# A three-block attention and mixture kernel on one core: new order of the steps inside an attention slot, masks behind both heads' scores, hi/lo splits as steps of their own

## What is computed

```python
# 1: attention, 8 heads of 64; heads 0-3 see the last 32 keys, heads 4-7 each 32nd key
scores = scale * q @ k.T ; masked ; attn = softmax(scores) ; x = attn @ v   # x: 576 x 512
# 2: token mixing and a channel layer
theta = x @ w_theta
yr = einsum('ts,bsd->btd', w_tok_r, x * cos(theta)) ; yi = the same with w_tok_i and sin
u = x + yr + yi ; x2 = u + relu(u @ w_ch)
# 3: 4 experts, top 2 by a gate, each a causal attention of one head
q, k, v = x2 @ wq[e], x2 @ wk[e], x2 @ wv[e]
out += gate[e] * (softmax(causal(q k.T)) @ v) @ wo[e]
```

## Time and profile before

| | us |
|---|---|
| median of 3 runs | 807.71 (800.57 to 808.68) |
| profiled execution | 807.49 |
| its span, first to last instruction | 805.7 |
| PE busy / DVE busy / ACT busy / POOL busy | 662.0 / 368.5 / 267.8 / 125.9 |
| one pass of BODY (third) | 193.7 |

### The profile page before, as it was taken

How to read it: one execution, slowest core, us unless ns; L and a number is a source line. 1 busy time by engine, 2 the same in 40 slices (tenths; PEclk the granted TensorE clock), 3 DMA queues, 4 the chain that set the end, 5 groups by cost and what they waited for, 6 DMA issues and landing times.

```text
span 805.7 us, 13113 instructions
## 1 busy us (share of the span) xinstructions
PE 662.0 (82%) x4469; PEld 535.7 (66%) x4469; DVE 368.5 (46%) x858; ACT 267.8 (33%) x791; POOL 125.9 (16%) x132
## 2 busy tenths in 40 slices
PE   3766798779888888787889879878888788997987
PEld 2654697768555588777655569767755558985654
DVE  2562755346546423355644633344554553334353
ACT  3461542453222441253421253044422145121222
POOL 1212330012201150012111133001120113100111
PEclk9695999999579998799866999889966899998769
DMA  7402044100000104200000011410000010000001
GB/s 237 116 18 78 11 99 99 31 16 16 1 1 0 53 9 109 50 4 20 8 1 1 27 34 35 94 31 15 18 1 0 1 40 21 1 1 1 1 1 59
DMA packets 73433, 27.33 MB, mean 34 GB/s; under 512 B 68624, under 2 KB 68624, under 8 KB 73360
## 3 DMA queue, kind: packets, MB, share of 16 engines
q1 hardware_dynamic: 70992, 22.70, 11.3%
q10 hardware_dynamic: 2368, 3.70, 1.2%
HBM read 21.67 MB, written 4.72 MB: 33 GB/s over the span
## 4 chain that ended last, share of the span: by engine, by line
PE 57%; issue 18%; DVE 10%; ACT 7%; POOL 4%; SPq 1%; DMA 1%; POOLq 0%; ACTq 0%; DVEq 0%
PE acc L1056 27%; PE wide L1056 11%; PE wide L1135 8%; PE turned L1170 4%; ACT probs L710 3%; POOL probs L648 2%; DVE xt L899 2%; PE turned L1155 2%; DVE probs L872 1%; ACT probs L718 1%; PE wide L1140 1%; DMA raw_k<-in_k 1%; PE wide L1116 1%; POOL probs L657 1%; DVE absf L914 1%
## 5 line engine op out<-in xcount | busy, mean ns | idle before, releaser
L727 ACT ACTIVATE pt<-turned 128x288 f32<-128x288 f32 (+5 forms) x72 | 30.8, 439 | 189.3 <-PE turned L1170 126.8
L1135 PE MATMUL wide<-k,q 64*128 64x128 f32 (+5 forms) x192 | 84.2, 592 | 0.6 <-DVE k L985 0.6
L1170 PE MATMUL turned<-ident,probs 128*128 128x128 f32 (+2 forms) x240 | 43.3, 324 | 41.6 <-DVE probs L872 26.4
L657 POOL TENSOR_TENSOR probs<-probs,weight 128x128 f32<-128x128 f32 (+4 forms) x40 | 31.5, 804 | 252.8 <-DVE weight L879 252.8
L840 DVE TENSOR_REDUCE nmax<-wide 128x1 f32<-128x128 f32 (+4 forms) x80 | 39.5, 537 | 56.8 <-PE wide L1140 56.7
L1170 PEld LDWEIGHTS turned<-ident,probs 128*128 128x128 f32 (+2 forms) x240 | 30.7, 172 | 50.6 <-DVE probs L872 24.5
L710 ACT ACTIVATE probs<-wide,nmax 96x128 f32<-96x128 f32 (+1 forms) x176 | 61.6, 379 | 5.7 <-DVE nmax L835 5.6
L1056 PE MATMUL wide<-w_tok_hi,z_hi 128*128 128x288 f32 x216 | 48.7, 307 | 11.1 <-POOL z_lo L673 11.1
L718 ACT ACTIVATE probs<-wide,nmax 128x128 f32<-128x128 f32 (+4 forms) x80 | 44.6, 573 | 26.0 <-DVE nmax L840 22.0
L666 POOL TENSOR_TENSOR xu_lo<-xt,xu_hi 128x576 fp32r<-128x576 f32 x16 | 22.5, 1403 | 162.3 <-ACT xu_hi L734 162.3
L1056 PE MATMUL wide<-w_tok_hi,z_lo 128*128 128x288 f32 x216 | 47.7, 303 | 0.0
(11 more groups left out here) (163 smaller groups left out, 1566.9 us busy)
## 6 DMA issues: line engine op xcount, KB each, us to landing
raw_q<-in_q SPq DMA_DIRECT2D x32, 128.0 KB, 2.4
raw_k<-in_k SPq DMA_DIRECT2D x32, 128.0 KB, 2.4
out<-o_sb SPq DMA_DIRECT2D x16, 256.0 KB, 2.0
raw_v<-in_v SPq DMA_DIRECT2D x64, 31.5 KB
raw_v<-in_v SPq DMA_DIRECT2D x16, 120.0 KB
raw_r<-in_moe_w_tok_r ACTq DMA_DIRECT2D x1, 1152.0 KB, 8.7
stage<-in_moe_w_theta ACTq DMA_DIRECT2D x2, 512.0 KB, 5.3
raw_i<-in_moe_w_tok_i ACTq DMA_DIRECT2D x1, 1024.0 KB, 10.5
```

Source lines behind the costliest of these rows:

```text
L657: ins = g.tensor_tensor(pr, pr, weight[0:rows, j:j + 1].broadcast_to([rows, t0 + rows]), ALU.mult)
L727: ins = a.activation(dst, src, ACT.Copy)
L1135: mm(wide[slot][0:rows, at0 + a0:at0 + a1], q3[hd, pr, t0:t0 + rows], k3[hd, pr, a0:a1], start=True, stop=True)
L1170: ins = nc.tensor.transpose(turned[slot][0:k, x:x + rows], probs[0:rows, hh, at0:at0 + k], ident[0:rows, 0:rows])
```

## The change

All of it is in the step lists and in what the steps emit.

1. A slot is laid out anew. With s1 work behind: `turn(b,0)`, `scores(a)`, `max(a,0)`, `turn(b,1)`, `max(a,1)`, `exp(a,0)`, gap 0, `values(b)`, `prep`, `norm(a,0)`, gap 1, `tail`, `exp(a,1)`, gap 2, `norm(a,1)`, `xu`, gap 3. With s3 work behind: `turn(b,1)` stands behind gap 0 and `values(b)` behind `exp(a,1)`.
2. The maxima are steps (`max`), the last 64 tokens of `prep` are a step (`tail`), and so are the splits of x (`xu`), of x2 (`x2hi`) and of z (`split`).
3. In s3 `scores` the masks of both heads stand behind the scores of both heads.
4. FILL has four gaps in a slot and other contents. `products` 0 and 1 and `split` 0 are ahead of the last two `out` steps.
5. `at_hi` and `at_lo` lie elsewhere in SBUF, clear of the chunks of z that `split` 0 writes.

```diff
@@ def attention_steps(units, before, fill):
         if behind:
             steps.append(("turn",) + behind + (0,))
         if ahead:
-            steps.append(("scores",) + ahead)
-        if behind:
+            steps += [("scores",) + ahead, ("max",) + ahead + (0,)]
+        if first:
             steps.append(("turn",) + behind + (1,))
+        if ahead:
+            steps += [("max",) + ahead + (1,), ("exp",) + ahead + (0,)]
         steps += gap[0]
+        if first:
+            steps.append(("values",) + behind)
+        elif behind:
+            steps.append(("turn",) + behind + (1,))
+        if nxt and nxt[0] == "s1":
+            steps.append(("prep",) + nxt)
         if ahead:
-            steps.append(("exp",) + ahead + (0,))
-        if not last_prep:
-            steps += prep
+            steps.append(("norm",) + ahead + (0,))
         steps += gap[1]
+        if nxt and nxt[0] == "s1":
+            steps.append(("tail",) + nxt)
         if ahead:
-            steps += [("norm",) + ahead + (0,), ("exp",) + ahead + (1,)]
-        if behind:
+            steps.append(("exp",) + ahead + (1,))
+        if behind and not first:
             steps.append(("values",) + behind)
         steps += gap[2]
         if ahead:
             steps.append(("norm",) + ahead + (1,))
+        if first:
+            steps.append(("xu", behind[1]))
+        steps += gap[3]
@@
-WAVE = [("products", 0), ("trig", 2), ("products", 1), ("wave", 0), ...
+WAVE = [("trig", 2), ("split", 1), ("products", 2), ("wave", 0), ("split", 2), ...
@@
 FILL = [
-    [channel(1), channel(2), channel(3)],
-    [halves("qk", 0), halves("qk", 2)[:1], halves("qk", 2)[1:]],
+    [channel(1), channel(2), x2(1) + halves("channel", 3)[:1], halves("channel", 3)[1:] + x2(2) + x2(3)],
+    [halves("qk", 0)[:1], halves("qk", 0)[1:], halves("qk", 2)[:1], halves("qk", 2)[1:]],
...
-BODY = [("load",)] + attention_steps(S1_UNITS + S3_UNITS, PREP + channel(0), FILL) + WAVE
+BODY = [("load",)] + attention_steps(S1_UNITS + S3_UNITS, PREP[:1] + channel(0) + PREP[1:] + x2(0), FILL) + WAVE
@@ s3 scores on PE
                             for hh, slot in enumerate(slots):
                                 hd = slice(hh * HD, (hh + 1) * HD)
                                 mm(wide[slot][0:rows, at0 + a0:at0 + a1], q3[hd, pr, t0:t0 + rows], k3[hd, pr, a0:a1],
                                    start=True, stop=True)
-                                if a1 == n:
-                                    part = slice(0, P) if rows == P else hd
-                                    ins = mm(wide[slot][0:rows, at0 + t0:at0 + n], ident_b[part, part],
...
+                        for hh, slot in enumerate(slots):
+                            part = slice(0, P) if rows == P else slice(hh * HD, (hh + 1) * HD)
+                            ins = mm(wide[slot][0:rows, at0 + t0:at0 + n], ident_b[part, part],
```

More of the change, by code:

```diff
@@ L52, in local, with z_chunks, attention_steps @@
     return p < PAIRS // 2
-def attention_steps(units, before, fill, last_prep=False):
+def z_chunks(m):
+    return (NT - 1,) if m == NT - 1 else (m, NT + m)
+def attention_steps(units, before, fill):
     steps = list(before)
@@ L64, in attention_steps @@
         behind = units[i - 1] if i else None
+        nxt = units[i + 1] if i + 1 < len(units) else None
         gap = list(fill[i]) if i < len(fill) else []
-        gap += [[]] * (3 - len(gap))
-        prep = [("prep",) + units[i + 1]] if i + 1 < len(units) and units[i + 1][0] == "s1" else []
+        gap += [[]] * (4 - len(gap))
+        first = bool(behind) and behind[0] == "s1"
         if behind:
@@ L127 @@
-PROLOGUE = attention_steps(S1_UNITS, PREP, SETUP, last_prep=True) + [("weights", 2)] \
-    + theta(0) + [("trig", 0)] + theta(1) + [("trig", 1)] + theta(2, 3, 4) \
+SETUP = [[[], [], [], [("piece", 0)]], [[], [("piece", 1)], [], [("wtok", ch) for ch in range(0, 2)]],
+         [[], [], [], [("wtok", ch) for ch in range(2, 6)]], [[], [], [], [("wtok", ch) for ch in range(6, ZC_N)]]]
+PROLOGUE = PREP + attention_steps(S1_UNITS, [], SETUP) + [("weights", 2)] \
+    + theta(0) + [("trig", 0), ("products", 0)] + theta(1) + [("trig", 1), ("products", 1)] + theta(2) + [("split", 0)] \
+    + theta(3, 4) \
@@ L151 @@
     [[], [], []],
-    [out_of(0), [], out_of(1)],
+    [[], out_of(0), out_of(1)],
     [out_of(2), [], out_of(3, 4)],
 ]
-EPILOGUE = attention_steps(S3_BY_PAIR, channel(0, 1, 2, 3) + halves("qk", 0, 2), FILL_LAST)
+EPILOGUE = attention_steps(S3_BY_PAIR, [x for o in range(KC) for x in channel(o) + x2(o)] + halves("qk", 0, 2), FILL_LAST)
 GATE_OPS = 12
@@ L187, in events @@
         return {f"qk_loaded{p % 2}": 16 * qk_dmas(p)}
[L188 to L189 removed]
+    if k == "max":
+        return {"negmax": 1}
     if k == "norm":
@@ L555, in emit @@
                         load_v(r, p)
-                elif kind == "prep" and step[2] < 2:
-                    wait_full(sp, "turned", uses[2])
+                elif kind == "tail" and step[2] < 2:
+                    wait_full(sp, "turned", uses[0])
                     load_qk(r, step[2] + 2)
@@ L659, in emit @@
                     ins.then_inc(s["probs_pool"], 1)
[L660 to L664 removed]
+                elif kind == "xu":
+                    p = step[1]
                     pool.wait_ge(s["xh"], c.at("xh", 1))
@@ L667, in emit @@
                         .then_inc(s["xl"], 1)
-                elif kind == "products":
+                elif kind == "split":
                     m = step[1]
@@ L1084, in emit @@
                         ins.then_inc(full["turned"][slot], 1)
-                    slot = free("turned", 2)
+                    note["prep"] = uses
+                elif kind == "tail":
+                    p = step[2]
+                    slot = free("turned", 0)
                     own()
@@ L1250, in emit @@
                     ins.then_inc(full["turned"][slot], 1)
-                    note[("zl", m)] = [c.at("zl", n + 1) for n in range(len(z_chunks(m)))]
+                elif kind == "split":
+                    note[("zl", step[1])] = [c.at("zl", n + 1) for n in range(len(z_chunks(step[1])))]
                 elif kind == "wave":
```

150 lines of the change are left out of this document (77 added, 73 removed).

## The result

The changed kernel takes **686.07 us** (median of 4 runs, 685.05 to 686.61), the kernel before in the same session 808.19 (800.57 to 813.65): a ratio of 0.8514 [0.8455, 0.8574]. The profiled execution took 685.98 us, its span is 684.2. The ratios leave out an execution that lies over 1.5% above the fastest of its kernel, which bears on experiments 1 to 4 (one run of the kernel before) and on experiment 6 (its own highest run, the profiled one).

What follows compares the result with a forecast made beforehand. PE was taken as the bound, busy 662 of 805.7 us. Three passes -78.5, set-up -5.5 and epilogue -8.5 gave 807.5 - 92.5 = 715 us, range 692 to 752.

Steps and rivals of the forecast that it cites:

- Parts 1 to 3: s1 slots: `tail` apart, POOL's order and slot 4's new layout remove PE waits, -14.3 us a pass.
- part 2: s1 slots: POOL scales head 1 ahead of splitting x, removing PE waits of 4.8 us in four places.
- Part 1: s1 slots: gap work between `prep` and `tail` removes PE's waits for q's copy, 10.7 us a pass.
- Part 4: s1 slots: less idle time gives more time at 2.4 GHz, -4 us a pass, bounds 0 and -9.
- Part 5: s3 scores: with masks behind both heads, the two heads run together on the array halves, -8.4 us a pass.
- rival B: Array halves don't overlap with 128 output columns, only the order changed: about 750 us; chance 0.17 together with A.
- Part 6: s3 slots, turn(b,1) behind `theta`: net 0; slots 8 to 10 to the first wave matmul: net 0.
- Part 7: Set-up: z_lo wait of 4.04 us goes and -1.5 in its slots, together -5.5; epilogue: masks and small terms, -8.5.
- A: Waits come back under other names, DVE queuing copies PE needs: about 755 us; chance 0.17 together with rival B.
- C: Denser slots keep the clock high in both s1 and s3 slots: about 676 us; chance 0.08.
- D: Slower than before: the chain exp(a,1), reciprocal, POOL, turn(a,1) bounds each s1 slot: about 822 us; chance 0.02.

Runs made afterwards that it cites:

- experiments 1 to 4: Kernel before with only the masks moved: 762.24 us; changed kernel with masks back: 724.02, with old s1 slots: 753.87, with `tail` right behind `prep`: 693.43.
- experiment 6: Changed kernel with the split of x (`xu`) ahead of POOL's scaling `norm(a,1)` again: 691.62 us, ratio 0.852.
- experiment 2: Changed kernel with each head's mask behind its own s3 scores again: 724.02 us, ratio 0.90.
- Experiment 10: Changed kernel with seven unread matmuls ahead of `values` in five s3 slots of each pass, where PE waits: 674.90 us, ratio 0.8346.
- experiment 1: Kernel before with only the s3 masks moved behind both heads' scores: 762.24 us, ratio 0.9462.
- experiments 8 and 9: Changed kernel with the old end of the set-up: 684.23 us; with the old order around the wave in both BODY and set-up: 693.18 us.

## Why the prediction missed

**Where the 29 us are.** The three passes gave 106.8 us where the sum had 78.5; the EPILOGUE 14.4 where it had 8.5; the set-up with its wave 0.3 where it had 5.5. That is 28 and 6 us more, and 5 less.

**Parts 1 to 3 (waits of the s1 slots, -14.3 a pass): right.** Idle time of the s1 slots in the third pass went from 17.5 to 2.8 us, and restoring them brought 45 us of idle time back against 43. Within them, part 2's mechanism (POOL's order) wasn't needed: undoing it alone changes nothing that can be told apart. Part 1's separate `tail` takes only 9.5 us of the 32.4 us wait for q's copy; the earlier `values` takes 4 more, and the later exp(a,1) and the new fill, which were not tried alone, must hold the rest. The delay of the lo splits of x2 beside POOL, which the prediction priced at up to 4.4 us, hardly came: in slot 0 of the third pass one split starts at 459.33 while POOL scales (458.20 to 459.67), and the longest of all 16 took 0.95 us, where 0.76 is usual. The `den` of the earlier trace rows reads one SBUF tile and not two, so it isn't the case of two inputs that the prediction names, though in all three passes before it lasted until POOL's split was done (1.02, 1.40, 1.40 us).

**Part 4 (clock in the s1 slots, "I take -4", bounds 0 and -9): this is the step that failed.** The mechanism was right, the size and the reach were not. The s1 slots have no low clock left at all, and their PE busy fell from 69.7 to 58.8 us with the same matmuls: -10.9 where the term had -4, and past its bound of -9. And the sum had no clock term for any other stretch. In the s3 slots PE busy fell by 12.1 (61.7 to 49.6), where the masks had 8.4; in the wave by 2.4, where the sum had nothing (0.95 to 1.00). These three make up the 13 us of PE busy a pass that the sum lacks, and the EPILOGUE (0.83 to 0.92) is of the same kind. My ground for -4 was that "low stretches also occur in busy places". That was a true reading with the wrong conclusion: experiment 2 shows such a busy place, and it is the one-head scores that the change itself removes. Experiment 10 shows that the clock is a cause of time and not a companion of it: nothing but the idle stretches was filled, and the kernel got 11 us faster.

**Part 5 (masks, -8.4 a pass, 33.5 in all): mechanism right, size too small.** 44 us by experiment 1 and 38 by experiment 2. The two heads overlap, so rival B fell. A unit takes 2.6 us, forecast 2.9, so the overshoot is mostly clock, not matmul time.

**Part 6 (net 0 a slot, net 0 around the wave): first half right, second off by up to 3 us.** `values` waits 2.05 to 2.40 us in five slots a pass, forecast 1.7 to 2.1, and undoing the move is even. The new order around the wave is worth some 3 us a pass (experiments 8 and 9).

**Part 7: the EPILOGUE (-8.5) gave 102.8 to 88.4, -14.4, the clock again. The set-up (-5.5) gave 0.3:** I removed the wait for z_lo and didn't ask what DVE holds up while it waits for ACT, and 4.09 us of waits came in its place. The other 1.5 us, in the set-up slots, didn't show either. The EPILOGUE's term was also added up wrongly: 8.3 + 0.7 - 1.1 is 7.9, not 8.5.

**Rivals.** A fell (idle time is down by 41 us). C came closest and named the missing term: 676 us, 10 below the measured time, where the forecast is 29 above it. Its price was too high for the s3 slots, which still had 10 us of low clock in the third pass, with the new wait for `pt`. Its chance of 0.08 was too small: all pieces of it were in the earlier trace rows. D was nowhere near.

## What to carry to other kernels

Where the granted clock is under 1.0, price a removed TensorE gap at more than its length: here about half as much again (45 us of waits, 24 of clock), and give that term to the stretches behind the gap as well. Look for stretches in which the engine counts as busy but does half-array work one head at a time, since here they cost clock like a gap (experiment 2). When two engines' work is interleaved by hand, move the instructions that nobody needs yet (here `theta`'s three on DVE) behind the copy that TensorE waits for: that was worth 36 us, where the whole change gave 122.

## What was not expected of the hardware

- Waits of 2.05 to 2.40 us, five a pass, go with three falls to 1.2 GHz in the first and the third pass (0.92 over 63.5 us is 10 us low) and with more in the second (0.87). In the third pass the low stretches begin at 522.9, 543.4 and 553.6, at the end of such a wait or up to 1.5 us behind it. Filling the waits with unread matmuls gave 1.00 in the first and third pass, 0.94 in the second, and 11 us in all.
- A fall can come with PE busy 6.00 of 6.00 us (experiment 2), in one-head scores with masks between. Both heads together take 0.92 us for 384 columns, one head alone 0.84 to its mask, so the second head is nearly free. The Trainium skill ("TensorEngine Tiling (Array Packing)", Key Properties) says that a change of tiling mode drains TensorE; the rows agree that half-array and full-array matmuls don't overlap here. That the clock falls in this alternation, three times in three passes, is shown by experiment 2; why it does stays open.
- The wave's matmuls went from 0.95 to 1.00 in experiment 1, where nothing around the wave was touched. Before, the clock is 1.00 ahead of the wave, PE waits 2.36 us for z_lo, and the fall comes 1.4 us into the wave, with PE busy; in experiment 1 the same wait of 2.36 us is followed by no fall. So a fall doesn't hang on the last wait alone, and what else it hangs on stays open.
